# First expert weights split into two f16 parts during attention, with factors on x rows, and a first product of three f16 products

## The reference, cut to what matters

```python
# attention: B, H, S, D = 4, 8, 768, 48, float32; k_n = k / (norm(k) + 1e-6)
for t in range(S):
    y[:, :, t] = q_t @ state
    state = state + beta_t * outer(kn_t, v_t - state^T kn_t)
# x = y as [3072, 384]; experts: E = 8, D = 384, F = 1024
logits = (x / (norm(x) + 1e-6)) @ en.T / tau
expert_idx = argmax(logits, axis=1)
gate_w = softmax(logits) at expert_idx
out[mask_e] = gate_w * (relu(x[mask_e] @ w1[e]) @ w2[e])
# dense: h = relu(out @ w_in) with F = 2048;  result = (h * h) @ w_out
```

## Time and profile before

| | |
|---|---|
| median of 3 runs | 1134.91 us (1131.6 to 1135.95) |
| the profiled execution | 1133.42 us, its span 1131.6 us (1.8 us lie around the span) |
| attention block | about 0 to 420 us; `first_t` runs 24 times, from 31.5 to 390.4 us |
| experts block | about 420 to 736 us; `up` of slot 0 begins at 421.39, `down` of slot 0 at 429.64, `down` of slot 30 at about 727.5 us |
| dense block | about 740 to 1131 us |
| busy over the span | PE 94%, weight loads 73%, DVE 60%, ACT 52%, POOL 28% |

### The profile page before, as it was taken

The page is one execution under the profiler, slowest core; times in us unless marked ns, Lnnn a source line. Parts: engine busy times, 40 slices in busy tenths (PEclk is TensorE's granted clock), DMA queues, the critical chain, the costliest instruction groups (busy, mean ns, idle before and its releaser), DMA issues. The chain is left out here.

```text
span 1131.6 us, 25343 instructions
## 1 busy us (share of the span) xinstructions
PE 1064.5 (94%) x10332; PEld 828.0 (73%) x10332; DVE 674.0 (60%) x1381; ACT 586.5 (52%) x1229; POOL 322.5 (28%) x292
## 2 busy tenths in 40 slices
PE   3799999999999879999999999879999999999998
PEld 1577888888887769999999999835555555555554
DVE  4788888888888626675557656634343434344333
ACT  2577677776777644555556656523332433333332
POOL 4466767777666632100002100041010100000000
PEclk9899999999999979999999999979999999999999
DMA  6122123332331055998656416131010100000000
GB/s 116 22 42 47 32 43 72 79 87 61 76 85 45 16 172 194 372 393 296 246 198 202 168 46 248 39 87 30 29 30 1 44 15 29 1 28 1 28 1 28
DMA packets 119091, 106.03 MB, mean 94 GB/s; under 512 B 78072, under 2 KB 108480, under 8 KB 118976
## 3 DMA queue, kind: packets, MB, share of 16 engines
q1 hardware_dynamic: 108976, 80.56, 23.9%
q0 software_dynamic: 5536, 17.50, 4.7%
q10 hardware_dynamic: 4464, 6.35, 1.5%
HBM read 129.90 MB, written 21.68 MB: 134 GB/s over the span
## 5 line engine op out<-in xcount | busy, mean ns | idle before, releaser
L1758 PE MATMUL mlp_ps<-xg_t,win 128*128 128x512 f16 x864 | 202.5, 382 | 1.0 <-DVE xg_t L1857 1.0
L1769 PE MATMUL mlp_ps<-wout,sq_hl 128*128 128x384 f16 x1128 | 197.0, 326 | 0.0
L1364 PE MATMUL expert_ps<-xs_t,w_sb 128*128 128x128 f32 x1488 | 173.7, 277 | 1.3 <-issue 0.6
L1364 PEld LDWEIGHTS expert_ps<-xs_t,w_sb 128*128 128x128 f32 x1488 | 172.7, 194 | 2.3 <-issue 1.4
L1769 PEld LDWEIGHTS mlp_ps<-wout,sq_hl 128*128 128x128 f16 x1128 | 110.4, 98 | 81.9
L1758 PEld LDWEIGHTS mlp_ps<-xg_t,win 128*128 128x128 f16 x864 | 85.0, 99 | 94.2 <-issue 2.8
L1864 DVE TENSOR_TENSOR sq<-relu 128x512 f32<-128x512 f32 x96 | 66.5, 693 | 138.6 <-ACT relu L1807 132.0
L1478 DVE TENSOR_TENSOR w_hl<-w_sb,w_hl 128x1536 fp32r<-128x1536 f32 x62 | 108.6, 1753 | 54.4 <-ACT w_hl L1413 54.4
L1375 PE MATMUL expert_ps<-w_hl,ht_hl 128*128 128x384 f32 x744 | 137.5, 339 | 0.6 <-issue 0.6
L839 DVE TENSOR_TENSOR p_cur<-newt,cst 128x256 f16<-128x256 f32 x288 | 109.0, 419 | 45.9 <-PE newt L453 42.5
L1807 ACT ACTIVATE relu<-mlp_ps 128x512 f32<-128x512 f32 x96 | 57.3, 597 | 147.4 <-PE mlp_ps L1758 147.4
(11 more groups left out here) (226 smaller groups left out, 1642.9 us busy)
## 6 DMA issues: line engine op xcount, KB each, us to landing
w_sb<-in_moe_w SPq DMA_DIRECT2D x62, 1536.0 KB
...
```

The lines of the kernel that those rows point to most:

```text
L1364: mm = pe.matmul(ps[:, 1 + half, c * P:(c + 1) * P], w1_sb[j % 2][:, kd, f], xs_t[:, kd], start=(kd == 0), stop=(kd == KD - 1))
L1758: mm = pe.matmul(ps[:, 4 + f % 2, :], win[:, a, kd, f * P:(f + 1) * P], xg_t[:, par, b, kd], start=(kd == 0 and a + b == 0), stop=(kd == K ...
L1769: mm = pe.matmul(ps[:, t, 0:DM], sq_hl[:, f % RING, a, t * P:(t + 1) * P], wout[:, b, f], start=(f == 0 and a + b == 0), stop=(f == K2 - 1 ...
```

## The change

Each chunk of w1 (8 experts by 3 chunks of 128x1024) is loaded twice during attention. The first copy is squared and summed on ACT (`square_weight`), summed over the partitions by PE (`weight_sum`), and DVE makes a rough inverse root from it by integer operations (`weight_factor`). The second copy is multiplied by the factor on DVE (`scale_weight`), rounded to f16 on ACT (`high_weight`), and the remainder is made on POOL (`low_weight`). Both parts go to a DRAM tensor `w1_hl`, and at the end the factors. A row of x gets a factor of its own (`x_factor` on DVE), ACT writes the scaled row to `x_all` (`scale_x`), and the factor travels as column 385 of `sorted_x`. In the experts, `up(j)` is 72 f16 products 128x128x128, x has a low part too (`low_x` on DVE), and the output's factor takes in both factors (`scale_back` and one more operation in `keep_y`). The diff, cut to its core:

```diff
+        def load_squared(i):
+            if not i < W_ALL:
+                return
+            if i >= KD:
+                sp.wait_ge(s_w_sq, i - W_RING + 1)
+                sp.wait_ge(s_w_sq_in, 16 * i)
+            e, kd = divmod(i, KD)
+            sp.dma_start(w_sq[:, i % W_RING], w1[e, kd * P:(kd + 1) * P, :]).then_inc(s_w_sq_in, 16)
+        def load_split(i):
+            if not i < W_ALL:
+                return
+            wait(sp, s_w_lo, i - KD + 1)
+            wait(sp, s_w_in, 16 * i)
+            e, kd = divmod(i, KD)
+            sp.dma_start(raw_chunk(i), w1[e, kd * P:(kd + 1) * P, :]).then_inc(s_w_in, 16)
+        def store_split(i):
+            if i < 0:
+                return
+            e, kd = divmod(i, KD)
+            cols = slice(kd * sh.F1 // 2, (kd + 1) * sh.F1 // 2)
+            sp.wait_ge(s_w_lo, i + 1)
+            wait(sp, s_w_out, 16 * i)
+            sp.dma_start(w1_hl[e][:, 0:sh.W1].rearrange("p (a c) -> p a c", a=2)[:, :, cols],
+                         rt.w1_sb[0][:, 0:sh.W1].rearrange("p (a c) -> p a c", a=2)[:, :, cols])\
+              .then_inc(s_w_out, 16)
 
...
+            if n == 3:
+                load_squared(3)
+            if n >= 3:
+                load_squared(n + 1)
+                load_split(n - 3)
+                store_split(n - 6)
             if n >= NP - FILLS:
                 clear(n - NP + FILLS)
+        for n in range(NP, NP + 6):
+            load_split(n - 3)
+            store_split(n - 6)
+        sp.wait_ge(s_w_factor, 3 * E)
+        sp.wait_ge(s_w_out, 16 * W_ALL)
+        sp.dma_start(w1_hl[:, :, sh.W1:sh.W1 + 2].rearrange("e p o -> p e o"), w_factor[:, :, :]).then_inc(s_w_out, 16)
         sp.wait_ge(rt.s_slots, 1)
         rt.scattered(sp, sh.EARLY)
         rt.load_x(sp, sorted_x, 0)
         e = rt.expert(sp, 0)
-        rt.load_w1(sp, w1, e, 0)
         rt.load_w2(sp, w2, e, 0)
+        sp.wait_ge(s_w_out, 16 * (W_ALL + 1))
+        rt.load_w1(sp, w1_hl, e, 0)
 
...
             difference(n - 1)
+            low_weight(n - 2)
             low_part(n - 1)
...
+        def low_weight(i):
+            if not 0 <= i < W_ALL:
+                return
+            pool.wait_ge(s_w_hi, i + 1)
+            pool.tensor_tensor(w_hl[:, 1, i % KD], raw_chunk(i), w_hl[:, 0, i % KD], ALU.subtract).then_inc(s_w_lo, 1)
...
+        def weight_sum(n):
+            if summed_in(n) is None:
+                return
+            e = summed_in(n)
+            if there(n - 2):
+                pe.wait_ge(s_xt, n - 1)
+            pe.wait_ge(s_w_sq, KD * (e + 1))
+            pe.matmul(y_ps[:, KD * P + E:KD * P + E + KD], cst[:, cs.ONES:cs.ONES + P], w_ss[:, KD * e:KD * (e + 1)],
+                      start=True, stop=True).then_inc(s_w_sum_ps, 1)
+        def weight_sum_read(n):
+            if summed_in(n) is not None:
+                pe.wait_ge(s_w_part, summed_in(n) + 1)
 
...
             newton_t(n, 2)
+            weight_sum(n)
             route(n - 2)
             if n == 0:
+                weight_sum_read(n)
...
             act.wait_ge(s_y_ps, n + 1)
             wait(act, s_ysq, n)
-            act.copy(y_tile[:, :], y_ps[:, 0:DM])
-            wait(act, rt.s_scatter[n % RING], 16 * (n // RING))
-            act.copy(x_all[:, n % RING, :], y_ps[:, 0:DM]).then_inc(s_y, 1)
+            wait(act, s_xall, n)
+            act.copy(y_tile[:, :], y_ps[:, 0:DM]).then_inc(s_y, 1)
+        def scale_x(n):
+            if not there(n):
+                return
+            act.wait_ge(s_xf, 2 * n + 2)
+            act.activation(x_all[:, n % RING, 0:DM], y_tile[:, :], ACT.Copy, scale=x_all[:, n % RING, DM:DM + 1])\
+               .then_inc(s_xall, 1)
+        def square_weight(n):
+            for i in squares_in(n):
+                act.wait_ge(s_w_sq_in, 16 * max(KD, i + 1))
+                wait(act, s_w_sq, i)
+                act.activation(w_junk[:, :], w_sq[:, i % W_RING], ACT.Square, accum_out=w_ss[:, i:i + 1])\
+                   .then_inc(s_w_sq, 1)
+        def keep_weight_sum(n):
+            if summed_in(n) is None:
+                return
+            e = summed_in(n)
+            act.wait_ge(s_w_sum_ps, e + 1)
+            wait(act, s_w_factor, 3 * e - 2)
+            act.copy(w_part[:, :], y_ps[:, KD * P + E:KD * P + E + KD]).then_inc(s_w_part, 1)
+        def high_weight(i):
+            if not 0 <= i < W_ALL:
+                return
+            act.wait_ge(s_w_scaled, i + 1)
+            wait(act, s_w_out, 16 * (i - KD + 1))
+            act.copy(w_hl[:, 0, i % KD], raw_chunk(i)).then_inc(s_w_hi, 1)
 
...
             keep_logits(n - 2)
+            keep_weight_sum(n)
+            square_y(n - 2)
             newton_t(n, 3)
             newton_tt(n, 3)
             store_turned(n + 1, 3)
+            high_weight(n - 1)
             newton_t(n, 4)
             square_k(n + 3)
             newton_tt(n, 4)
             store_turned(n + 2, 0)
             newton_t(n, 5)
             newton_tt(n, 5)
-            square_y(n - 2)
+            scale_x(n - 2)
             newton_tt(n, 6)
             if n == 0:
                 keep_emb()
...
                 keep_beta()
             high_rhs(n)
             store_turned(n + 2, 1)
+            square_weight(n)
 
...
+        def x_factor(n):
+            if not there(n):
+                return
+            def step(ins):
+                ins.then_inc(s_xf, 1)
+                dve.wait_ge(s_xf, 2 * n + 1)
+            dve.wait_ge(s_ysq, n + 1)
+            wait(dve, s_xf, 2 * n)
+            wait(dve, rt.s_scatter[n % RING], 16 * (n // RING))
+            inverse_root(dve, step, x_all[:, n % RING, DM:DM + 1], x_shift[:, :], ssx[:, n:n + 1], X_PART)\
+                .then_inc(s_xf, 1)
+        def weight_factor(n):
+            if summed_in(n) is None:
+                return
+            e = summed_in(n)
+            def step(ins):
+                ins.then_inc(s_w_factor, 1)
+                dve.wait_ge(s_w_factor, 3 * e + 2)
+            if e == 0:
+                dve.wait_ge(s_zero, 2)
+            dve.wait_ge(s_w_part, e + 1)
+            dve.tensor_reduce(w_total[:, e:e + 1], w_part[:, :], AX.X, ALU.add).then_inc(s_w_factor, 1)
+            dve.wait_ge(s_w_factor, 3 * e + 1)
+            inverse_root(dve, step, w_factor[:, e, 0:1], w_shift[:, e:e + 1], w_total[:, e:e + 1], W_PART)\
+                .then_inc(s_w_factor, 1)
+        def scale_weight(i):
+            if not 0 <= i < W_ALL:
+                return
+            e, kd = divmod(i, KD)
+            dve.wait_ge(s_w_factor, 3 * e + 3)
+            dve.wait_ge(s_w_in, 16 * (i + 1))
+            dve.tensor_scalar(raw_chunk(i), raw_chunk(i), w_factor[:, e, 0:1], None, ALU.mult).then_inc(s_w_scaled, 1)
 
...
             lead(n - 2, 0)
+            scale_weight(n - 1)
             newton_p(n, 4)
             new_values(n - 1)
             store_products(n + 1, 3)
             newton_p(n, 5)
             new_state(n - 1)
+            x_factor(n - 2)
+            weight_factor(n)
             sum_k(n + 3)
             newton_p(n, 6)
             store_products(n + 2, 0)
...
-                    for kd in range(KD):
-                        mm = pe.matmul(ps[:, 1 + half, c * P:(c + 1) * P], w1_sb[j % 2][:, kd, f], xs_t[:, kd],
-                                       start=(kd == 0), stop=(kd == KD - 1))
+                    for a, b in ((0, 0), (1, 0), (0, 1)):
+                        for kd in range(KD):
+                            mm = pe.matmul(ps[:, 1 + half, c * P:(c + 1) * P], w1_hl_sb[j % 2][:, a, kd, f], xs_hl[:, b, kd],
+                                           start=(a + b + kd == 0), stop=(b == 1 and kd == KD - 1))
...
-            act.copy(xs_t[:, :, :], ps[:, 0, 0:DM].rearrange("p (k t) -> p k t", k=KD)).then_inc(s_xt, 1)
+            act.copy(xs_hl[:, 0], ps[:, 0, 0:DM].rearrange("p (k t) -> p k t", k=KD)).then_inc(s_xt_hi, 1)
 
...
+        def low_x(j):
+            dve.wait_ge(s_xs[j % 2], 16 * (j // 2 + 1))
+            wait(dve, s_y_scale, j - 1)
+            dve.tensor_copy(x_scale[:, j % 2:j % 2 + 1], xs[j % 2][:, DM:DM + 1]).then_inc(s_x_scale, 1)
+            dve.wait_ge(s_xt_hi, j + 1)
+            dve.tensor_tensor(xs_hl[:, 1], ps[:, 0, 0:DM].rearrange("p (k t) -> p k t", k=KD), xs_hl[:, 0],
+                              ALU.subtract).then_inc(s_xt, 1)
+        def scale_back(j):
+            dve.wait_ge(s_x_scale, j + 1)
+            dve.wait_ge(s_w1[j % 2], 16 * (j // 2 + 1))
+            wait(dve, s_ys, j - 1)
+            dve.tensor_tensor(y_scale[:, j % 2:j % 2 + 1], x_scale[:, j % 2:j % 2 + 1], rt.w1_factor(j % 2), ALU.mult)\
+               .then_inc(s_y_scale, 1)
...
-            factor = ys[:, j % 2, DM:DM + 1]
+            factor = y_factor[:, :]
             step(inverse_root(dve, step, factor, shifted[:, 0:1], y_ss[:, j % 2:j % 2 + 1], dense.PART))
+            dve.wait_ge(s_y_scale, j + 1)
```

(4 more changed lines are left out.)

115 lines of the change are left out of this document (86 added, 29 removed).

## The result

The kernel with the change takes 1143.85 us (median of 7 runs, 1141.68 to 1149.17), the kernel before in the same sessions 1135.48 us (7 runs, 1131.6 to 1138.32). The ratio is 1.0092, with a 95% interval from 1.0064 to 1.012: slower by nearly 1%, and 2 us under the forecast of 1146. As a difference it is 8.4 us by the medians and 10.4 by the ratio. The profiled execution took 1148.05 us, one of the two longest.

What follows compares the result with a forecast made beforehand. It took PE to bound the experts, and the waits among PE, DVE and ACT to set attention's pass. From the profiled execution, 1133.4 - 18 + 26 + 1 + 4.5 = 1146.9, forecast as 1146 us; own range 1137 to 1157.

Steps and rivals of the forecast that it cites:

- Experts: Expert slots: shorter `up` cuts the period from 9.87 to 9.13 us; 18 us saved in all, bounds 0 and 33.
- The chain: Experts, ACT and DVE steps on the `w2_hl` half buffers from one `down` to the next: 8.98 + 0.15 = 9.13 us.
- The 81 ns: Experts' `up`: the skill's spacing for 128-column products with weight loads, giving 5.8 us; the prediction took 4.1 us instead.
- The loss to DMA: Experts: eight successive slots with fresh weights need 9.4 us of DMA, losing 0.2 each, 1.5 us in all.
- Attention: Attention loop: 1.2 us added in 21 passes, 0.35 in the three after; 26 us in all, bounds 5 and 42.
- The lock between POOL and VectorE: Attention: VectorE's small `norm_k` operations wait out POOL's `low_weight`; booked at 0.3 us per pass.
- Seam: Between attention and experts: last `low_weight`, stores and loads delay w1 of slot 0; 4.5 us added, bounds 0 and 10.
- Start: Ahead of the first attention pass: three squares and 1.6 MB more in the first loads; 1 us added.
- attention absorbs it: Rival, attention: slack takes up late hand-overs, leaving 0.2 us per pass; total 1126 us, chance 0.19.
- PE stays the bound: Rival, experts: the ACT and DVE steps have unseen slack, slots take 8.6 us; total 1133, chance 0.08.
- More exclusion between POOL and VectorE: Rival, attention: the two engines block each other more often, `scale_weight` costs in full; 2.0 us per pass, 1163, chance 0.13.
- Open weight loads: Rival, experts' `up`: weight loads aren't hidden, 7.1 us replace 5.4, 31 slots lose 1.7 each; 1217 us, chance 0.04.

Runs made afterwards that it cites:

- e_up1: The changed kernel with only the 24 high-part products of the experts' first product, the 48 with a low part left out: 1180.19 us, single run.
- e_xfac: The changed kernel with `x_factor` and `weight_factor` on VectorE moved from behind `new_state` to ahead of `newton_p` of level 5: 1136.06 us, ratio 1.0019 to the kernel before.
- e_sqmove: The changed kernel with `square_weight` on ScalarE moved from ahead of `keep_x1` to ahead of the last `newton_tt`: 1145.34 us, ratio 1.0085 to the kernel before.
- e_half_low: The changed kernel with `low_weight` on POOL done on only the first half of the chunk's columns: 1136.83 us, ratio 1.0025 to the kernel before.
- e_two_lows: The changed kernel with `low_weight` on POOL cut into two halves, both computed, the second behind `norm_k`: 1138.98 us, ratio 1.003 to the kernel before.
- e_few_scaled: The changed kernel with `scale_weight` on VectorE done on 64 of the chunk's 1024 columns: 1140.12 us, ratio 1.005 to the kernel before.
- e_xs: The changed kernel with the moves of e_xfac and e_sqmove together: 1137.34 us, ratio 1.0025 to the kernel before.
- e_x_two: The changed kernel with the edits of e_xfac and e_two_lows together: 1132.97 us, ratio 0.9985 to the kernel before.
- e_chain: The changed kernel with the second half of `low_w2` moved on VectorE behind `low_h` of its own slot's first half: 1149.91 us, ratio 1.0155 to the kernel before.

## Why the prediction was right

The time and the sign were right, and most of the mechanisms. That the sum came so near is partly luck, for its terms were off by up to 5 us in both directions: 5 too little saved in the experts, 5 too little lost at the seam, and in attention a price per pass that was too high beside falls of the clock that weren't booked. The starting value helped too. The sum, 1146.9, is 13.5 us above an execution that was faster than the median, and was then rounded down to 1146; the measured difference is 8.4 to 10.4 us.

*Experts, 18 us forecast, 22 measured, and 1.0 more in slot 0.* f16 products of 128 columns at 57 ns, 4.1 us: measured 56 ns, 4.03 us. The chain at 9.13 us: measured 9.08, and e_up1 shows that ScalarE and VectorE set it. PE waits 0.30 us before `down`, not 0.5. Mis-sized were several small terms, by the distances from `down` to `down` in both traces: ordinary slots saved 0.81 us and not 0.74 (1.7 us in all), slots 1, 2 and 6 saved 0.65 each and not 0.2 (1.4), slot 3 saved 0.1 and didn't lose 0.4. The loss to DMA, booked at 1.5 us, can't be seen: slots 7 and 8, with the DMA share at 1.04 to 1.05 from 530 to 550, took 9.07 and 9.08 like all others. Against this, slot 4 lost 1.4 us by the clock. The 81 ns of the Trainium skill (TensorE: Matmul & The Clock Gate, Back-to-back issue gap), which the prediction weighed, would have given an `up` of 5.8 us, an estimate; these rows decide against it.

*Attention, 26 us forecast, 29 in the profiled execution, 21 to 23 in the three others with the same code.* Of its parts:

- `x_factor` and `weight_factor`, booked at 0.35 + 0.2 us a pass, 12 us: e_xfac won 8, and 0.25 a pass where the clock is full. Right in place and nearly in size.
- `square_weight`, booked at 0.5 us a pass, some 10 us: undisturbed passes got 0.3 shorter in e_sqmove, but no time was won. This step was wrong in its path and too large. x1 does come later, but `apply_a` wasn't waiting for it alone: of x1's 0.33 us, 0.07 reach it. The prediction read 251.31 as right behind x1, and x1 had been there since 251.02.
- The lock between POOL and VectorE, booked at 0.3 us on the two `tensor_tensor` operations of `norm_k`: e_half_low and e_two_lows won 8 and 7 us, 0.3 a pass. The size was right, the victim was another: the first `tensor_scalar`, which waits 0.64 us longer.
- `scale_weight`, booked at 0 because its idle time would hide it: e_few_scaled won 5 us, 0.13 a pass. This step failed. The prediction asked only who waits on VectorE and PE and not on POOL, which the operation holds up. For its duration the prediction had the choice between 1.15 us from a row and 0.6 from the Trainium skill (VectorE: DVE Perf Modes, Mode 2x_2P): by itself it takes 0.74, so the Trainium skill was nearer; what the profile shows on average, 1.16, is waiting.
- The clock isn't in the prediction at all. It took its share of the long passes, and the uniform 1.2 us that I forecast is really 0.7 us in the ordinary pass and the rest in a few passes of 18 to 19. So the 16.7 to 17 us a pass that were to show the forecast right are met only by the mean, 16.9; the median is 16.4.

The single gains (8, 7, 5) add up to nearly what attention lost, and so do those per undisturbed pass: 0.25 + 0.28 + 0.13 = 0.66 of 0.75. Overlaps such as those of e_xs and e_x_two show that such sums needn't close.

*Seam, 4.5 us forecast, 9.5 measured.* This was the worst term. Stores and loads came in the order forecast, and the last `low_weight` ended 23.1 us behind the last `first_t`, where 22.6 were forecast. But the loads took 11.0 us and not 8.3, with those of slot 1 beside them, and I let them run partly beside the second store, while x, w2 and w1 are all issued behind the last chunk's store and come 3.5 us after the issue of the factors'. The bound, 10, held.

*Start, 1 us forecast:* -0.8.

Rivals: that attention absorbs it (1126) is refuted, passes lost 0.7 us and not 0.2. That PE stays the bound and slots go to 8.6 is refuted, though the eleven short periods of e_chain lie near the 8.6 that the prediction gave PE. More exclusion between POOL and VectorE was partly true: both waits exist, but the pass lost a third of the 2.0 us. Open weight loads are refuted.

What stays open: which stretch of attention lets the clock fall in one execution and not in the next. The attention code of the change has shown 7, 8, 12 and 30 low microseconds in four executions. Open too is by which path the square costs what it does.
